# A two-chunk-first order for the attention preprocessing of a fused mixer and MLP kernel

## The chip, the cores and the metric

The kernel runs on one core of one Trainium2 chip. The metric is the device time of one execution in microseconds; several executions are timed and the median is quoted. The engines are called PE (TensorE), DVE (VectorE), ACT (ScalarE), POOL (GpSimd) and SP (SyncE, which here only issues DMAs). Each runs its own program strictly in order and waits on semaphores.

## The reference

Three stages follow each other. The first is linear attention with a complex decay per feature, the second an MLP with a hard-swish, the third a gated MLP.

```
mag   = sqrt(a_re^2 + a_im^2);  scale = min(mag, 0.999) / (mag + 1e-6)
S[t]  = a[t] * scale[t] * S[t-1] (complex) + k[t] (outer) v[t]
y[t]  = q[t] . Re(S[t])                          # 4 batches, 8 heads, 768 tokens, 48 features
h = y @ w_in;   g = h * clip(h + 3, 0, 6) / 6;   x2 = g @ w_out            # 3072 x 384 x 2048
out = ((x2 @ w1) * (x2 @ w2)) @ w3 @ w_out2                                # 384 x 1024 x 384
```

Everything is float32. The two MLPs use split products: each operand is written as a high part and a low part, and three matmuls replace one.

## The kernel before

**Tiling.** The 3072 tokens are cut into 24 chunks of 128 tokens, three to a unit, so there are 8 units of 384 tokens (`NU = 8`, `CPU = 3`). A batch is two units; the last of its six chunks carries no state on. The first MLP walks a unit in 16 *slots*, one per tile of 128 hidden features (`FT1 = 16`). Slot n has the matmuls of `gemm1` for hidden tile n (L796, into `hb`) and those of `gemm2` for tile n-2 (L816, into `acc`). Between them a tile goes through four engine steps: ACT adds 3 and clips below (`t_sb`, "relu", L1046), DVE forms the hard-swish (`g_sb`, L1237), ACT copies its high part (`gH`, `high_g`, L1036), POOL subtracts to get the low part (`gL`, L1328). `g_sb` and `t_sb` are single buffers, so the relu of a slot waits for the hard-swish of the slot before and the hard-swish for the low part of the slot before. Units run from -2 to 7; units -2 and -1 have no MLP and only prepare.

**What runs beside it.** While unit u is in the MLP, the attention of unit u+1 is done chunk by chunk and the decays of unit u+2 are computed. Three tables say in which slot what stands.

- `steps(u, sl)` gives the preprocessing steps `t = 0..15` of a unit p ("the chain") that ACT and DVE do in a slot; for u of 1 and more, step t of p = u+2 stands in slot t. The chain works in place on `AR`, `AI` and three work tiles `W1`, `W2`, `W3` (all 128 x 1152). It takes logarithm, magnitude, arctangent and running sums of the decays, then multiplies q and k by the exponentials of the sums ("products", L1170 and L1183, into `QKs`) and by cosine and sine ("rotation", L1198 into `QKc`, L1202 into `QKs`).
- `chunk(u, sl, stage)` gives the attention. In units of 1 and more, TK (transposes of k, L832) stands in slots 1, 5, 9, S (scores, L846) in 2, 6, 10, and YU (the output y and the state product, L865 to L878) in 4, 8, 12. After TK, ACT and DVE copy k out (L1059 to L1061, L1249 to L1251). After S, DVE masks the scores (L1260). After YU, ACT takes y's high part (L1067), DVE its low part (L1266) and adds to the state `Z` (L1218, L1221), decaying it for the next chunk (L1228).
- `W3_COPY`, `SPLIT_H` and `SPLIT_L` place the copies of the product w3 times w_out2 and the splitting of the first MLP's weights in the early units.

**SP's queue.** All transfers but five are issued by SP, in program order. `load_a` (L640) fetches `AR` and `AI` for the next p. `load_q` and `load_k` (L651, L656) fetch q and k for all three chunks of p. `scatter_pair` (L338 to L342; "sorting") moves the rotated rows of the first two chunks from `QKc` and `QKs` into head order in `F`, five DMAs for each source; `scatter_last` (L670) does it for the third chunk, once the first chunk's YU has freed the buffer. `store_x` (L707 to L712) sends y as the MLP's input `xHL`, in six DMAs, after DVE's low part of y. For p = 0 ACT issues the second five DMAs of `scatter_pair`.

Within a slot, the order on an engine matters below. ACT: relu, (in slot 1 the two copies L409 of the previous unit's result), the chain's step, `high_g`, the copies after TK, y's high part. DVE: hard-swish, the chain's step, the copies after TK, masks, y's low part and the state. SP: `scatter_last`, `load_v`, `store_x`, `load_q`, `load_k`, then what the chain's step asks for (`load_a` at t = 12, `scatter_pair` at 14 and 15).

At the end of unit 7 the second MLP's weights are split, each in one piece: ACT's copies in slots 4, 6, 8 (L1081), DVE's subtractions in 5, 7, 9 (L1279). After the last unit comes the second MLP (L937, L959), which the change does not touch.

## Time and profile before

| | us |
|---|---|
| median of the timed runs (3) | 1017.98 |
| lowest and highest of them | 1017.22 and 1024.38 |
| the profiled execution's own time | 1022.37 |
| its span, first to last instruction | 1020.6 |
| PE busy in the span | 910.4 |
| DVE, ACT, POOL busy | 470.5, 430.5, 256.6 |

The span is what the profile shows; 1.8 us lie around it. Units 0 to 7 of the first MLP run from about 101 us to 707 us. PE's busy time is nearly the span, so what counts are the places where it idles and the stretches in which its clock is low. A slot can be followed by ACT's relu (L1046): one stands in each slot, 128 in all.

### The profile page before, as it was taken

What the parts mean: (1) busy time and instruction counts of PE and PEld (TensorE: products, weight loads), DVE (VectorE), ACT (ScalarE), POOL (GpSimd) and SP (SyncE); (2) the same over time, 40 slices, a digit from 0 to 9 for tenths busy, and PEclk for the clock granted to TensorE, in tenths of its full rate; (3) what the DMA queues carried; (4) which work ended last, traced back from release to release, by engine and by line L of the source; (5) the groups of instructions that cost most, each with busy time, mean ns of one, the idle gap of its engine ahead of it and who ended that gap; (6) DMA issues with size and microseconds to landing.
All of it is one profiled execution on the core that took longest, in us unless ns stands there. A gap on an engine that the chain in (4) does not pass through costs nothing.

```text
span 1020.6 us, 14665 instructions
## 1 busy us (share of the span) xinstructions
PE 910.4 (89%) x5721; PEld 834.9 (82%) x5721; DVE 470.5 (46%) x610; ACT 430.5 (42%) x650; POOL 256.6 (25%) x200
## 2 busy tenths in 40 slices
PE   6944469889989989989989989989999999999996
PEld 3534468879889889889889889989888888888886
DVE  6445549849658648648748733233212121212110
ACT  4543535555655655555555532353212122212121
POOL 1011336222222222222222222343222222222221
PEclk9977769989989999999999999999999999999999
DMA  9584132353343343343344141510101010101000
GB/s 347 201 230 128 46 63 78 85 119 88 108 87 95 100 91 98 93 90 99 107 89 110 48 84 50 188 68 11 44 1 62 1 62 1 62 1 62 1 32 33
DMA packets 73688, 85.85 MB, mean 84 GB/s; under 512 B 6928, under 2 KB 59792, under 8 KB 73616
## 3 DMA queue, kind: packets, MB, share of 16 engines
q1 hardware_dynamic: 73216, 84.07, 29.7%
q10 hardware_dynamic: 400, 0.80, 0.5%
q8 instruction: 48, 0.79, 0.3%
q14 instruction: 24, 0.20, 0.1%
HBM read 45.22 MB, written 11.01 MB: 55 GB/s over the span
## 4 chain that ended last, share of the span: by engine, by line
issue 39%; PE 38%; POOL 14%; DVE 3%; ACT 2%; DMA 2%; SPq 1%; ACTq 0%; POOLq 0%; DVEq 0%
POOL gL L1328 13%; PE hb L937 10%; PE acc L959 7%; PE bQ L937 5%; PE bR L937 5%; PE bP L959 2%; PE hb L796 2%; PE acc L816 2%; PE acc L890 2%; DMA F<-QKs 1%; PE hb L890 1%; DVE QKc L1198 1%; DMA wo_sb<-in_moe_w_out_dram 1%; PE bQ L846 0%; PE bR L846 0%
## 5 line engine op out<-in xcount | busy, mean ns | idle before, releaser
L1328 POOL TENSOR_TENSOR gL<-g_sb,gH 128x384 fp32r<-128x384 f32 x128 | 157.1, 1227 | 428.2 <-ACT gH L1036 425.9
L796 PE MATMUL hb<-xHL,winH 128*128 128x384 f32 x768 | 168.6, 356 | 10.7 <-DMA xHL<-yHL 9.1
L816 PE MATMUL acc<-gH,woutH 128*128 128x384 f32 x384 | 134.0, 349 | 32.5 <-POOL gL L1328 23.6
L1237 DVE SCALAR_TENSOR_TENSOR g_sb<-t_sb,hb 128x384 f32<-128x384 f32 x128 | 70.4, 550 | 189.6 <-ACT t_sb L1046 105.8
L796 PEld LDWEIGHTS hb<-xHL,winH 128*128 128x128 f32 x768 | 140.2, 199 | 13.3 <-DMA xHL<-yHL 9.5
L1046 ACT ACTIVATE t_sb<-hb,cst 128x384 f32<-128x384 f32 x128 | 74.4, 581 | 154.1 <-PE hb L796 153.4
L816 PE MATMUL acc<-gH,woutL 128*128 128x384 f32 x384 | 133.3, 347 | 0.0
L816 PE MATMUL acc<-gL,woutH 128*128 128x384 f32 x384 | 132.8, 346 | 0.0
L1341 POOL TENSOR_TENSOR pL<-p_sb,pH 128x512 fp32r<-128x512 f32 x48 | 67.0, 1396 | 231.9 <-ACT pH L1098 231.9
L816 PEld LDWEIGHTS acc<-gH,woutH 128*128 128x128 f32 x384 | 75.0, 195 | 37.6 <-issue 29.3
L1036 ACT CAST gH<-g_sb 128x384 fp32r<-128x384 f32 x128 | 65.3, 510 | 79.4 <-DVE g_sb L1237 79.2
L796 PE MATMUL hb<-xHL,winL 128*128 128x384 f32 x384 | 88.9, 339 | 0.0
L816 PEld LDWEIGHTS acc<-gH,woutL 128*128 128x128 f32 x384 | 75.4, 196 | 0.0
L816 PEld LDWEIGHTS acc<-gL,woutH 128*128 128x128 f32 x384 | 75.2, 196 | 0.0
L1090 ACT COPY a_sb<-hb 128x512 f32<-128x512 f32 x48 | 28.1, 586 | 102.7 <-PE hb L937 102.7
L796 PEld LDWEIGHTS hb<-xHL,winL 128*128 128x128 f32 x384 | 70.4, 192 | 0.0
L1296 DVE TENSOR_TENSOR p_sb<-a_sb,bQ 128x512 f32<-128x512 f32 x24 | 16.5, 688 | 110.2 <-PE bQ L937 94.4
L1098 ACT CAST pH<-p_sb 128x512 fp32r<-128x512 f32 x48 | 29.8, 621 | 85.5 <-DVE p_sb L1296 85.5
L1296 DVE TENSOR_TENSOR p_sb<-a_sb,bR 128x512 f32<-128x512 f32 x24 | 16.5, 686 | 104.7 <-PE bR L937 99.7
L846 PE MATMUL bQ<-F 128*128 128x128 f32 x192 | 32.5, 323 | 28.2 <-DMA F<-QKs 26.8
L846 PEld LDWEIGHTS bQ<-F 128*128 128x128 f32 x192 | 29.3, 228 | 31.9 <-DMA F<-QKs 29.7
L959 PE MATMUL acc<-woH,pL 128*128 128x384 f32 x144 | 48.7, 338 | 0.0
(148 smaller groups left out, 1715.9 us busy)
## 6 DMA issues: line engine op xcount, KB each, us to landing
QKs<-in_qk_x_dram SPq DMA_DIRECT2D x16, 576.0 KB, 4.2
xHL<-yHL SPq DMA_DIRECT2D x48, 144.0 KB, 2.7
F<-QKc SPq DMA_DIRECT2D x16, 292.5 KB, 4.7
AR<-in_a_re_x_dram SPq DMA_DIRECT2D x8, 576.0 KB, 3.9
AI<-in_a_im_x_dram SPq DMA_DIRECT2D x8, 576.0 KB, 4.8
v_sb<-in_v_dram SPq DMA_DIRECT2D x24, 192.0 KB, 2.5
x_dram<-x_sb SPq DMA_DIRECT2D x24, 192.0 KB, 4.1
out_dram<-o_sb SPq DMA_DIRECT2D x6, 768.0 KB, 4.3
```

The lines of the kernel that those rows point to most:

```text
L796: mm = pe.matmul(o, w[:, kk * DF1 + ft * P:kk * DF1 + (ft + 1) * P], xv(u)[:, 2 * kk + part, :], start=(i == 0), stop=(i == 8))
L816: mm = pe.matmul(acc[m][:, 0:UNIT], w[:, ft * DM + m * P:ft * DM + (m + 1) * P], gg[:, (n % 3) * UNIT:(n % 3 + 1) * UNIT], start=(ft == 0 ...
L846: mm = pe.matmul(bk[:, hh * P:(hh + 1) * P], qk(f_of(g))[:, b, P:2 * P], qk(f_of(g))[:, b, 0:P], start=True, stop=True)
L890: mm = pe.matmul(w3_banks[i % nb][:, 0:DM], w3t_sb[:, j * DF2 + i * P:j * DF2 + (i + 1) * P], wo2_sb[:, j * DM:(j + 1) * DM], start=(j == ...
L937: mm = pe.matmul(bk[n % 2][:, :], w[:, kk * DF2 + ft * P:kk * DF2 + (ft + 1) * P], x[:, o:o + UNIT2], start=(i == 0), stop=(i == 8))
L959: mm = pe.matmul(acc2[tb][:, 0:DM], pp[:, o:o + P], w[:, ft * DM:(ft + 1) * DM], start=(ft == 0 and i == 0), stop=(ft == FT2 - 1 and i == 2))
L1036: act.copy(gH[:, (n % 3) * UNIT:(n % 3 + 1) * UNIT], g_sb[:, :]).then_inc(s["hswish_high"], 1)
L1046: act.activation(t_sb[:, :], hb[n % 2][:, 0:UNIT], ACT.Relu, bias=THREE_C).then_inc(s["relu_done"], 1)
L1237: dve.scalar_tensor_tensor(out=g_sb[:, :], in0=t_sb[:, :], scalar=6.0, in1=hb[n % 2][:, 0:UNIT], op0=ALU.min, op1=ALU.mult).then_inc(s["hs ...
L1296: dve.tensor_tensor(p_sb[:, (n % 2) * UNIT2:(n % 2 + 1) * UNIT2], a_sb[:, (n % 2) * UNIT2:(n % 2 + 1) * UNIT2], bb[n % 2][:, :], ALU.mult) ...
L1328: pool.tensor_tensor(gL[:, (n % 3) * UNIT:(n % 3 + 1) * UNIT], g_sb[:, :], gH[:, (n % 3) * UNIT:(n % 3 + 1) * UNIT].bitcast(F32), ALU.subt ...
L1341: pool.tensor_tensor(pL[:, (n % 3) * UNIT2:(n % 3 + 1) * UNIT2], p_sb[:, (n % 2) * UNIT2:(n % 2 + 1) * UNIT2], pH[:, (n % 3) * UNIT2:(n % ...
```

## The change

It rewrites the chain's last steps and moves several others.

- q and k are loaded in two pieces, chunks 0 and 1 of a unit (`load_pair`, issued at TK of the second chunk) and chunk 2 (`load_last`, at TK of the third), where it was q and then k.
- Products and rotation are done for the two first chunks (t = 10 and t = 12) and later for the third (t = 13 and t = 14). Six full-width instructions become twelve: six of two thirds, six of one third.
- DVE's sums move from t = 7 and 11 to t = 6 and 9, the arctangent's product from 8 to 7. ACT's exponentials and arctangent stand together at t = 8 (were 9 and 10), the turns at 10 (was 12), sine and cosine with their table loads at 11 (was 13).
- ACT's `high_g` stands ahead of the chain's step in a slot (and ahead of the copies L409), where it stood behind it.
- `scatter_pair` is issued at t = 12, both halves, and always by SP; `load_a` at t = 13, waiting for the last products.
- The tables of the early units move: the w3 copies earlier or later, the weight splits in another order, and the chain's steps of units 1 and 2 by one slot.
- The second MLP's weights are split in six halves, in slots 3 to 8 (ACT) and 4 to 9 (DVE), and their loads are issued two slots earlier.

```diff
-                return ([(1, 0)] if sl == 0 else []) + ([(1, sl + 1)] if sl < 9 else [])
+                return {0: [(1, 0), (1, 1)]}.get(sl, [(1, sl + 1)] if sl < 10 else [])
...
-            return [(u + 2, sl)] if u + 2 < NU else []
+            if u == 1 and sl < 2:
+                return [(3, 0), (3, 1)] if sl else []
+            return [(u + 2, sl)] if u + 2 < NU and sl < 15 else []
...
-                    sp.wait_ge(s["k_decayed"], p)
+                    sp.wait_ge(s["last_decayed"], 2 * p)
...
                     for p, t in steps(u, sl):
-                        if t == 12 and p + 1 < NU:
+                        if t == 12:
+                            scatter_pair(sp, p, 0)
+                            scatter_pair(sp, p, 1)
+                        if t == 13 and p + 1 < NU:
                             load_a(p + 1)
-                        if t == 14:
-                            scatter_pair(sp, p, 0)
-                        if t == 15 and p > 0:
-                            scatter_pair(sp, p, 1)
...
                         act.activation(t_sb[:, :], hb[n % 2][:, 0:UNIT], ACT.Relu,
                                        bias=THREE_C).then_inc(s["relu_done"], 1)
+                        high_g(n)
                         if sl == 1 and u > 0:
                             evac_x2_act(act, u - 1)
-                    if n is not None:
                         for p, t in steps(u, sl):
                             pre(p, t)
-                        high_g(n)
...
+                if t == 12:
+                    dve.wait_ge(s["pair_decayed"], 2 * (p + 1))
                     dve.wait_ge(s["cos_turns"], p + 1)
                     for i in range(2):
-                        dve.tensor_tensor(part(QKc, i), part(QKs, i), tokens(W3), ALU.mult).then_inc(s["cos_rotated"], 1)
-                if t == 15:
+                        dve.tensor_tensor(pair(part(QKc, i)), pair(part(QKs, i)), pair(tokens(W3)), ALU.mult).then_inc(s["pair_cos"], 1)
                     dve.wait_ge(s["sin_turns"], p + 1)
                     for i in range(2):
-                        dve.tensor_tensor(part(QKs, i), part(QKs, i), tokens(W2), ALU.mult).then_inc(s["sin_rotated"], 1)
+                        dve.tensor_tensor(pair(part(QKs, i)), pair(part(QKs, i)), pair(tokens(W2)), ALU.mult).then_inc(s["pair_sin"], 1)
+                if t == 13:
+                    dve.wait_ge(s["last_dma"], 16 * (p + 1))
+                    for i, grow in enumerate((AI, AR)):
+                        dve.tensor_tensor(last(part(QKs, i)), last(part(QKs, i)), last(tokens(grow)), ALU.mult).then_inc(s["last_decayed"], 1)
...
-                    if u == NU - 1 and sl in (4, 6, 8):
-                        i = sl // 2 - 2
+                    if u == NU - 1 and 3 <= sl < 9:
+                        i, part2 = divmod(sl - 3, 2)
                         act.wait_ge(s[f"mlp2_w_dma{i}"], 16)
-                        act.copy(w2parts[i][0][:, :], w2parts[i][2][:, :]).then_inc(s["mlp2_w_high"], 1)
+                        act.copy(half(w2parts[i][0], part2), half(w2parts[i][2], part2)).then_inc(s["mlp2_w_high"], 1)
```

**Place 1: SP at the end of a unit (u from 1 to 4).** The last DMAs of `store_x`, then what stands before the next unit. Before:

```order
L711 DMA xHL<-yHL 16x2x128
L712 DMA xHL<-yHL 16x2x128
L640 DMA AR<-in_a_re_x_dram 128x1152
L640 DMA AI<-in_a_im_x_dram 128x1152
L338 DMA F_68<-QKc 48x2x780
L339 DMA F_68<-QKc 48x2x780
L340 DMA F_68<-QKc 32x2x520
L341 DMA F_68<-QKc 16x2x260
L342 DMA F_68<-QKc 16x2x260
L338 DMA F_68<-QKs 48x2x780
```

And with the change:

```order
L722 DMA xHL<-yHL 16x2x128
L345 DMA F_68<-QKc 48x2x780
L346 DMA F_68<-QKc 48x2x780
L347 DMA F_68<-QKc 32x2x520
L348 DMA F_68<-QKc 16x2x260
L349 DMA F_68<-QKc 16x2x260
L345 DMA F_68<-QKs 48x2x780
L346 DMA F_68<-QKs 48x2x780
L347 DMA F_68<-QKs 32x2x520
L348 DMA F_68<-QKs 16x2x260
L349 DMA F_68<-QKs 16x2x260
L647 DMA AR<-in_a_re_x_dram 128x1152
```

The ten DMAs of `scatter_pair` have moved from behind the loads of `AR` and `AI` to ahead of them.

**Place 2: ACT in slots 8 to 10 of such a unit, chunk 1's y among them** (`W_63`, `W_64`, `W_65` are `W1`, `W2`, `W3`). Before, from slot 8's relu:

```order
L1046 ACTIVATE t_sb<-hb,cst 128x384
L1036 CAST gH<-g_sb 128x384
L1067 CAST yHL<-bP 128x4x128
L1046 ACTIVATE t_sb<-hb,cst 128x384
L1013 ACTIVATE AI<-AR 128x1152
L1014 ACTIVATE AR<-AR 128x1152
L1036 CAST gH<-g_sb 128x384
L1046 ACTIVATE t_sb<-hb,cst 128x384
L1017 ACT_TABLE_LOAD
L1017 ACTIVATE W_64<-W_64 128x1152
L1036 CAST gH<-g_sb 128x384
```

And with the change:

```order
L1052 ACTIVATE t_sb<-hb,cst 128x384
L1042 CAST gH<-g_sb 128x384
L1022 ACTIVATE AI<-AR 128x1152
L1023 ACTIVATE AR<-AR 128x1152
L1025 ACT_TABLE_LOAD
L1025 ACTIVATE W_64<-W_64 128x1152
L1072 CAST yHL<-bP 128x4x128
L1052 ACTIVATE t_sb<-hb,cst 128x384
L1042 CAST gH<-g_sb 128x384
```

The exponentials, the table load and the arctangent, spread over slots 9 and 10 before, now stand in slot 8 ahead of y's high part. (Before, `mid_decay`, L1010, stands between the first two rows.)

**Place 3: ACT around sine and cosine.** Before, in slots 12 and 13:

```order
L1036 CAST gH<-g_sb 128x384
L1067 CAST yHL<-bP 128x4x128
L1046 ACTIVATE t_sb<-hb,cst 128x384
L1023 ACTIVATE W_65<-W_63 128x1152
L1025 ACT_TABLE_LOAD
L1025 ACTIVATE W_65<-W_65,cst 128x1152
L1026 ACTIVATE W_64<-W_63 128x1152
L1027 ACT_TABLE_LOAD
L1036 CAST gH<-g_sb 128x384
```

And with the change, in slots 11 and 12:

```order
L1052 ACTIVATE t_sb<-hb,cst 128x384
L1042 CAST gH<-g_sb 128x384
L1031 ACTIVATE W_65<-W_63 128x1152
L1033 ACT_TABLE_LOAD
L1033 ACTIVATE W_65<-W_65,cst 128x1152
L1034 ACTIVATE W_64<-W_63 128x1152
L1035 ACT_TABLE_LOAD
L1052 ACTIVATE t_sb<-hb,cst 128x384
L1042 CAST gH<-g_sb 128x384
L1072 CAST yHL<-bP 128x4x128
```

The block of five has moved from behind the last y's high part (slot 12) to ahead of it, and the high part of its own slot now stands ahead of the block.

## Rows read from the trace of the kernel before

**Rows 1.** Page, parts 1 and 2: busy times, and the granted clock by slices.

```profile
PE 910.4 (89%) x5721; PEld 834.9 (82%) x5721; DVE 470.5 (46%) x610; ACT 430.5 (42%) x650; POOL 256.6 (25%) x200
...
PEclk9977769989989999999999999999999999999999
```

**Rows 2.** Waits of PE: engine line, released by, us in total, times, longest.

```profile
PE bQ L846 <- DMA F<-QKs: 26.8, 8, 9.1
PE acc L816 <- POOL gL L1328: 23.6, 10, 8.0
...
PE acc L816 <- ACT gH L1036: 6.9, 5, 2.1
```

**Rows 3.** Timeline of PE, stalls at the starts of units 4 and 5: start, us.

```profile
428.65 0.52 PE L816 MATMUL acc<-gH,woutH 128*128 128x384 f32 x1 [2.10 <-POOL gL L1328]
...
445.94 2.08 PE L846 MATMUL bQ<-F 128*128 128x128 f32 x8 [2.72 <-DMA F<-QKs]
...
503.35 0.41 PE L816 MATMUL acc<-gH,woutH 128*128 128x384 f32 x1 [2.37 <-POOL gL L1328]
```

**Rows 4.** Windows of 1 us at an earlier boundary: length, PE, PEld, DVE, ACT, POOL, PEclk, DMA.

```profile
293.00:294.00 1.00, 1.00 (x5) 1.00 (x4) 0.62 (x4) 0.98 (x1) 0.85 (x1) 0.50 1.06 128
298.00:299.00 1.00, 1.00 (x7) 1.00 (x6) 0.69 (x1) 0.00 (x0) 0.00 (x0) 0.50 0.08 16
```

**Rows 5.** Timeline of ACT, slots 13 and 14 of unit 4.

```profile
494.77 0.58 ACT L1046 ACTIVATE t_sb<-hb,cst 128x384 f32<-128x384 f32 x1 [1.11 <-PE hb L796]
495.52 1.17 ACT L1023 ACTIVATE W<-W 128x1152 f32<-128x1152 f32 x1 [0.16 <-DVE W L1188]
...
501.62 0.51 ACT L1036 CAST gH<-g_sb 128x384 fp32r<-128x384 f32 x1
```

**Rows 6.** Timeline of ACT in plain slots of unit 7: the pitch of slots.

```profile
656.78 0.58 ACT L1046 ACTIVATE t_sb<-hb,cst 128x384 f32<-128x384 f32 x1 [1.40 <-PE hb L796]
...
659.90 0.58 ACT L1046 ACTIVATE t_sb<-hb,cst 128x384 f32<-128x384 f32 x1 [0.29 <-PE hb L796]
```

**Rows 7.** Timeline of DVE in slot 8 of unit 4.

```profile
474.94 0.55 DVE L1237 SCALAR_TENSOR_TENSOR g_sb<-t_sb,hb 128x384 f32<-128x384 f32 x1
...
478.76 0.68 DVE L1266 TENSOR_TENSOR yHL<-bP,yHL 128x512 fp32r<-128x512 f32 x1
```

**Rows 8.** Groups by line, chain work of ACT and DVE: shapes, count, busy us, mean ns.

```profile
L1178 DVE TENSOR_TENSOR_SCAN W<-W,total,W 128x384 f32<-128x384 f32 x12 | 14.1, 1230 | 0.2 <-ACT W L1017 0.2
...
L1198 DVE TENSOR_TENSOR QKc<-QKs,W 128x1152 f32<-128x1152 f32 x16 | 28.3, 1807 | 6.9 <-ACT W L1025 6.9
...
L1017 ACT ACT_TABLE_LOAD x8 | 10.3, 1283 | 0.1
...
L1013 ACT ACTIVATE AI<-AR 128x1152 f32<-128x1152 f32 x8 | 9.3, 1162 | 1.0 <-DVE W L1146 1.0
```

**Rows 9.** Timeline, last y of unit 4's attention and SP's issues behind it.

```profile
495.60 0.68 DVE L1266 TENSOR_TENSOR yHL<-bP,yHL 128x512 fp32r<-128x512 f32 x1
...
500.27 0.53 SPq L640 DMA_DIRECT2D AR<-in_a_re_x_dram  x1
```

**Rows 10.** Timeline of SP, first and last of the ten DMAs of the pair.

```profile
432.54 0.60 SPq L338 DMA_DIRECT2D F<-QKc  x1
...
440.62 0.59 SPq L342 DMA_DIRECT2D F<-QKs  x1
```

**Rows 11.** DMA issues by line: KB each, us from issue to landing.

```profile
AI<-in_a_im_x_dram SPq DMA_DIRECT2D x8, 576.0 KB, 4.8
```

**Rows 12.** Timeline of PE, stalls before and in unit 0.

```profile
62.54 2.08 PE L846 MATMUL bQ<-F 128*128 128x128 f32 x8 [9.05 <-DMA F<-QKs]
...
123.02 0.66 PE L816 MATMUL acc<-gH,woutH 128*128 128x384 f32 x1 [8.03 <-POOL gL L1328]
```

**Rows 13.** Timeline of PE and group of ACT, the second MLP's weights in unit 7.

```profile
684.93 0.66 PE L816 MATMUL acc<-gH,woutH 128*128 128x384 f32 x1 [2.38 <-POOL gL L1328]
...
L1081 ACT CAST w2H<-w_raw 128x3072 fp32r<-128x3072 f32 x1 | 2.8, 2769 | 0.0
```

More of the change, by code:

```diff
@@ L259, in rows_of, with half @@
             return t[:, :].rearrange("p (c j n) -> p j c n", j=KT, n=QK)
+        def half(t, i):
+            n = N1 // 2
+            return t[:, i * n:(i + 1) * n]
         def hd(t):
@@ L753, in _ @@
                         load_x2(0)
-                    if u == NU - 2 and sl == 15:
+                    if u == NU - 2 and sl == 13:
                         for i in range(2):
@@ L1274, in _ @@
                             pre(p, t)
-                    if u == NU - 1 and sl in (5, 7, 9):
-                        i = (sl - 5) // 2
-                        hi, lo, raw = w2parts[i]
-                        dve.wait_ge(s["mlp2_w_high"], i + 1)
-                        dve.tensor_tensor(lo[:, :], raw[:, :], hi[:, :].bitcast(F32), ALU.subtract).then_inc(s["mlp2_w_low"], 1)
+                    if u == NU - 1 and 4 <= sl < 10:
+                        i, part2 = divmod(sl - 4, 2)
+                        hi, lo, raw = (half(w_, part2) for w_ in w2parts[i])
+                        dve.wait_ge(s["mlp2_w_high"], sl - 3)
+                        dve.tensor_tensor(lo, raw, hi.bitcast(F32), ALU.subtract).then_inc(s["mlp2_w_low"], 1)
             split_x2_dve(dve, 0)
```

117 lines of the change are left out of this document (58 added, 59 removed).

## The prediction

> **What bounds the kernel now.** I read the page first. PE is busy for 910.4 of 1020.6 us and its granted clock is full from the middle on; in the first 23 of 40 slices it dips again and again, and DVE (470.5) and ACT (430.5) are far from full over the span [rows 1]. So PE bounds, and what can be won are its idle 110 us and what the low clock adds to them. PE's waits name the causes: 26.8 us for the sorted rows of F, 23.6 for POOL's low part, 6.9 for ACT's high part [rows 2]. The timeline of PE places them. From unit 1 on they come once a unit: about 2.1 for the low part, then 2.7 for F [rows 3]; just behind such stalls the granted clock is 0.50, the 1.2 GHz level, while PE is busy the whole of each window, at one boundary from 293 to 299 [rows 4]. A unit takes 503.35 - 428.65 = 74.7 us [rows 3].
>
> The first of the two comes from ACT: in slot 13 it does its relu and then the chain's five instructions from 495.52 on, 6.1 us, before the high part at 501.62 [rows 5]. A plain slot is 659.90 - 656.78 = 3.12 us [rows 6], and a tile has two slots from hidden to its second matmul. The second comes from DVE's rotation in slots 14 and 15 and the ten DMAs behind it. Together with the clock I put a boundary's loss at 5.5 + 3.3 = 8.8 us: six windows at half clock are 3 us of lost work.
>
> **The change, part by part.** The cycle of a unit closes through one event, DVE's low part of the last y. I call its end T: 495.60 + 0.68 = 496.28 in unit 4 [rows 9]. Before, the first scores of a unit start at 445.94, T comes 50.3 later, and from T to the next first scores it is 74.7 - 50.3 = 24.4 us [rows 3, 9].
>
> *From T to the scores.* Six DMAs of `store_x` take SP from T to 500.27, 4.0 us [rows 9]. Then, with the change, come the ten DMAs of the pair, 440.62 + 0.59 - 432.54 = 8.7 us [rows 10], and only behind them AR and AI, 0.5 for the first and 4.8 from AI's issue to landing [rows 11]: T + 18.0. ACT waits for this in slot 0 of the next unit (the squares, t = 0) and holds back all behind it: two squares 2.1, the relu of slot 1 0.5, DVE's hard-swish 0.5, the high part 0.5, the copies of the old unit's result 0.9. That is T + 22.5. PE's second matmuls of the new unit need those copies, 1.6, so the scores start at T + 24.1, against T + 24.4. The wait for F itself is gone (its rows land at about T + 17.5), but a wait for AR and AI takes its place. That part gives nothing.
>
> On what the ten DMAs cost SP, the 8.7 us are this trace's. The Trainium skill, DMA: Bandwidth & Descriptors, section "Issuing engines are not separate DMA queues", says that issuing from several engines only saves the sequencer's time to initiate, "which is usually small relative to the DMA itself". Here it is not small: 8.7 us of issue against about 5 to landing. By the page AR and AI would be little behind T + 9, the squares would wait for nothing, and about 8 us a unit would come off; I go by the row.
>
> *From the scores to T.* Three things come later. (1) Sine and cosine with their two table loads now stand in slot 11, behind that slot's high part but ahead of slot 12's relu. From their start: 6.1 [rows 5], relu 0.5, hard-swish 0.55 [rows 7], the pair's rotation, 4 instructions at two thirds of 1.81 [rows 8] = 4.8, y's low part 0.7: T is 12.6 later. With slot 11's high part on its own time (slot 13's relu at 494.77 [rows 5], less two slots of 3.1 and 5.1, plus 1.6: 488.1) T would be 500.7: 4.5 later than 496.28. (2) But it won't be on time. DVE's running sums, 3 x 1.23 [rows 8] and 1.3 for centring, move ahead of slot 6's masks, and make slot 8's hard-swish about 1.8 late. In slot 8 ACT now does two exponentials (2.1), a table load (1.28) and the arctangent (1.2), 4.6 us [rows 8], ahead of y's high part, while DVE stands at y's low part. That starts 0.55 + 0.5 + 4.6 + 0.6 = 6.2 behind the hard-swish, at 474.94 + 1.8 + 6.2 = 483.0; it was at 478.76 [rows 7], so 4.2 late. (3) From there DVE has no gap: 1.8 for y and the state, 0.55, the other sums 4.1, 0.55, the pair's products and the rounding 5.0, masks 1.4, 0.55, and ACT's high part 0.5: 497.4 in place of 488.1. T is then 497.4 + 12.6 = 510.0, 13.7 late. I take 11.5 a unit, since each link was taken at its full length, with 4.2 (nothing late but (1)) and 14 as ends. In the slots from 9 to 16 PE stalls in pieces: for the masks (2 us), for slot 12's hard-swish (3 to 4), for slot 13's behind the rotation (2), for the input `xHL` (1 to 2); in odd units slot 9's transposes wait for the state (up to 4).
>
> So the high part's own move wins the 2.1 us that it is meant to, and the chain behind it costs more. Four units (1 to 4) have both ends of this: 4 x 11.5 = +46. Unit 5 has no load of AR and AI behind it; T is 12 late, but the scores start when F has landed and PE has got there, T + 17.5 rather than T + 24.4: +5 (ends -3 and +8).
>
> *The early part.* The rotated pair of p = 0 is done some 5.5 us earlier, because the arctangent no longer stands behind a w3 copy. SP alone issues its ten DMAs, 4.4 us more than two queues side by side, and AR and AI for p = 1 come behind them, so the first scores' 9.05 us wait [rows 12] shrinks but masks wait for the chain: unit 0 begins 0 to 5.5 us earlier, I take 3. In unit 0 the stall of 8.03 us for the high part [rows 12] falls to about 5 (the chain still sits before the next relu), and the rotation is a slot earlier; I take 9.5 by slot 5, less 2.5 at the start of unit 1, where AR and AI are late again. Together -10, ends -20 and 0.
>
> *Unit 7.* The copies of 2.77 us become halves of 1.4, which fit in a slot of 3.12 beside 1.1 of relu and high part [rows 6, 13]. Slots 3 to 15 last 44.1 us where 12 x 3.12 = 37.4 are due; the 2.38 us stall is one of three [rows 13]. I take -5.5, ends -6.7 and 0.
>
> Splitting six instructions in twelve costs nothing to speak of: one third by itself is 0.55 as the hard-swish of the same width [rows 7], three of them 1.65 against 1.81 [rows 8].
>
> *Sum.* 46 + 5 - 10 - 5.5 = +35.5 on the profiled execution's 1022.4 us (span 1020.6 and 1.8 around it) is 1057.9. The median of the runs is 4.4 lower, so 1053.5; I say 1053.
>
> **The rivals.**
>
> *DVE keeps up.* If ACT's block in slot 8 falls in time that DVE has to spare (it is busy for under half of the span [rows 1], and some gap stands in each slot before), only (1) is left: 4 x 4.2 = 17, unit 5 about -3, and -15.5 for the early part and unit 7: -1.5, that is 1016. What decides is whether y's low part in slot 8 starts within 1 us of where it did. Against it: DVE's gaps in the middle of a unit before are about 9 of 44 us, and ACT's block alone takes half of them.
>
> *It does what it looks meant to.* AR and AI arrive in time, F's rows too, and the high part never waits. That would be if SP gets to the pair's DMAs early, ahead of `store_x`'s wait; for it speaks that F's wait is the largest row [rows 2] and that the rotation is two slots earlier. Against it: in SP's order the pair stands behind the last `store_x`, so an earlier rotation alone brings nothing. Price: 5 boundaries x 8.8 = -44, the early part -18, unit 7 -5.5: 950; with half of the boundaries' gain and the early part as forecast 980. It decides if T comes no later than before and AR and AI land within 10 us of it.
>
> *Worse.* The same mechanism with the low clock on top: PE stalls of 2 to 4 us follow each other from slot 9 to slot 2 of the next unit, and half clock over 10 us more in each of four units is 5 us each, with the early part at its bad end: 1053 + 20 + 10 = 1083. It decides if the clock stays at 0.5 in most of these slots.
>
> **How the numbers follow.** Forecast (1030 to 1075) 0.52, DVE keeps up (1003 to 1024) 0.18, as meant (945 to 1000) 0.22, worse 0.08. A measurement of this kernel tells about 1% from no change, 10 us. As meant is all faster; of the second case 0.04 is faster, 0.11 within 1%, 0.03 slower; the forecast and the worse case are slower. That gives faster 0.26, same 0.11, slower 0.63. The range leaves out the worse case and a little over half of the third case: 985 to 1077; the forecast's own range is 1030 to 1075.
>
> **What would show it.** In the new trace: AR's issue about 12.7 us behind the last y's low part, and in ACT's timeline the squares ending its longest idle time, on the load; PE waiting for `acc`'s copies or `Kc` at the start of units 2 to 5, no longer for F; y's high part in slot 8 starting right behind the arctangent, and DVE idle there for 5 us; units of about 86 us between first scores, against 74.7; unit 7 with no stall over 1 us. Wrong would be units under 74 us, squares that wait for nothing, or DVE idle in slots 9 to 11.

## The result and the profile after

| | before | changed | ratio (95% interval) |
|---|---|---|---|
| median of 4 runs each, us | 1017.6 | 1091.55 | 1.071 (1.066 to 1.076) |
| span of the profiled execution, us | 1020.6 | 1090.0 | |

The changed kernel is 7% slower, 74 us. The forecast had the sign and about half of the size (+35.5), and the measured time lies outside its range.

The page of the changed kernel, parts 1 and 2, the same rows as [rows 1]:

```profile
PE 925.9 (85%) x5721; PEld 846.0 (78%) x5721; DVE 483.6 (44%) x661; ACT 431.2 (40%) x653; POOL 254.3 (23%) x200
...
PEclk9966889869979988898987999999999999999999
```

PE has the same 5721 matmuls as before, so its 15.5 us more are the lower clock: there are more slices below 9 than in [rows 1], and they reach further, to slice 22 where it was 12. The other 54 us are idle time of PE. Its waits (engine line, released by, us in total, times, longest), against [rows 2]:

```profile
PE acc L826 <- ACT x_sb L416: 44.5, 5, 11.8
PE bQ L856 <- ACT Kc L1066: 22.8, 3, 12.9
PE hb L806 <- DVE g_sb L1249: 22.6, 10, 5.6
...
PE bQ L856 <- DMA F<-QKs: 6.3, 2, 5.5
...
PE acc L826 <- POOL gL L1340: 1.0, 1, 1.0
```

Both large rows of before are gone, F's from 26.8 to 6.3 and the low part's from 23.6 to 1.0. Larger ones stand in their place: five times PE waits for ACT to empty `acc`. The waits of all engines say what ACT and DVE are waiting for:

```profile
ACT gH L1042 <- DVE g_sb L1249: 205.4, 128, 6.7
DVE g_sb L1249 <- ACT t_sb L1052: 203.7, 51, 15.2
...
ACT W L995 <- DMA AI<-in_a_im_x_dram: 67.9, 8, 12.0
DVE yHL L1278 <- ACT yHL L1072: 47.4, 16, 5.7
```

The first row turned out to be the one that I had not thought of. Before, the first two read:

```profile
DVE g_sb L1237 <- ACT t_sb L1046: 105.8, 49, 8.6
...
ACT gH L1036 <- DVE g_sb L1237: 79.2, 82, 4.1
```

ACT now waits for DVE in every one of the 128 slots, where it did in 82. DVE waits for ACT about as often as before, 51 times, but for twice as long.

**A ruler for all runs.** ACT does one relu in each of the 128 slots. In its timeline the starts of the relus of slots 3 and 15 cut a unit in two: inside (slots 3 to 15) and boundary (slot 15 to slot 3 of the next unit, which holds the first scores; T lies ahead of slot 15's relu, by 8 to 9 us in the kernel before and by 3.4 to 4.0 in the changed one). For unit 3 of the changed kernel:

```profile
419.22 0.58 ACT L1052 ACTIVATE t_sb<-hb,cst 128x384 f32<-128x384 f32 x1 [1.87 <-PE hb L806]
...
480.77 0.58 ACT L1052 ACTIVATE t_sb<-hb,cst 128x384 f32<-128x384 f32 x1
...
508.56 0.58 ACT L1052 ACTIVATE t_sb<-hb,cst 128x384 f32<-128x384 f32 x1 [1.32 <-PE hb L806]
```

That is 61.6 inside and 27.8 at the boundary. Read so from the profile of each kernel (u0 is unit 0; "inside" and "boundary" are means over units 1 to 4; all in us):

| kernel | u0 slot 3 at | u0 inside | u0 to u1 | inside | boundary | u5 to u6 | u7 inside |
|---|---|---|---|---|---|---|---|
| before | 124.7 | 73.7 | 27.3 | 53.8 | 21.1 | 20.9 | 44.1 |
| changed | 128.0 | 82.6 | 28.9 | 60.9 | 29.0 | 16.6 | 37.5 |
| e1_a_ahead | 128.8 | 82.6 | 28.8 | 60.9 | 23.0 | 16.8 | 37.4 |
| e2_y_ahead | 129.0 | 85.0 | 31.0 | 59.8 | 25.8 | 15.6 | 37.4 |
| e5_both | 128.6 | 85.9 | 25.0 | 60.1 | 19.9 | 14.9 | 37.5 |
| e6_old_split | 124.1 | 84.5 | 28.4 | 61.0 | 28.9 | 16.8 | 37.5 |
| e8_early | 127.1 | 80.4 | 27.7 | 61.0 | 28.8 | 16.7 | 37.4 |
| e7_late_high | 127.6 | 77.0 | 29.0 | 57.0 | 28.8 | 16.8 | 37.4 |
| e12_ahead_late_high | 127.6 | 79.0 | 29.5 | 57.1 | 22.5 | 16.8 | 37.4 |
| e10_three | 128.5 | 84.0 | 25.6 | 60.2 | 19.3 | 15.6 | 37.5 |
| e14_spread | 127.0 | 77.1 | 29.1 | 55.1 | 18.8 | 20.5 | 37.4 |
| e15_spread_all | 127.0 | 70.0 | 27.6 | 55.1 | 18.8 | 18.9 | 37.5 |
| e16_spread_all_split | 123.7 | 69.6 | 26.7 | 55.1 | 18.7 | 20.3 | 37.5 |
| e3_before_high_first | 126.8 | 77.0 | 28.6 | 57.4 | 20.2 | 21.3 | 45.7 |
| e18_high_13 | 126.7 | 73.6 | 27.1 | 54.3 | 20.1 | 20.7 | 45.6 |
| e4_before_u7 | 126.7 | 73.3 | 27.2 | 53.8 | 20.3 | 21.1 | 37.4 |

A unit is 15.0 us longer: 7.1 inside, 7.9 at the boundary. Cut at T instead, it is 11.9 up to T and 3.2 behind it. Unit 0 and what is ahead of it lose 13.8 (3.3 + 8.9 + 1.6), unit 5 with its boundary 2.6, and the last unit wins 6.6. The pieces were taken apart one by one. The ruler has an error of its own: e4_before_u7 is the kernel before in all that runs ahead of unit 6's end, and yet its unit 0 is 2.0 us later and its boundary 0.8 shorter.

### The profile page after: what moved, and what is told of

Same layout as the page of the kernel before. It is cut to its first block, busy times and chain, and to the rows that moved or that the text cites. A ratio compares the mean times of both kernels' runs of the same rounds, so it can differ in the third digit from the quotient of the medians.

```text
span 1090.0 us, 14722 instructions
## 1 busy us (share of the span) xinstructions
PE 925.9 (85%) x5721; PEld 846.0 (78%) x5721; DVE 483.6 (44%) x661; ACT 431.2 (40%) x653; POOL 254.3 (23%) x200
## 3 DMA queue, kind: packets, MB, share of 16 engines
q1 hardware_dynamic: 64400, 84.87, 28.4%
## 4 chain that ended last, share of the span: by engine, by line
PE 48%; DVE 16%; issue 13%; SPq 8%; ACT 7%; DMA 6%; POOL 2%; DVEq 0%; ACTq 0%; POOLq 0%
PE hb L947 9%; PE acc L969 7%; PE acc L826 7%; PE hb L806 7%; DMA AI<-in_a_im_x_dram 5%; PE bR L947 4%; PE bQ L947 4%; PE bP L969 2%; SPq L347 2%; DVE g_sb L1249 2%; PE acc L900 2%; POOL gL L1340 2%; DVE W L1143 1%; DVE W L1126 1%; PE bQ L856 1%
## 5 line engine op out<-in xcount | busy, mean ns | idle before, releaser
L1340 POOL TENSOR_TENSOR gL<-g_sb,gH 128x384 fp32r<-128x384 f32 x128 | 152.9, 1194 | 497.5 <-ACT gH L1042 467.9
L806 PE MATMUL hb<-xHL,winH 128*128 128x384 f32 x768 | 173.4, 363 | 31.7 <-DVE g_sb L1249 22.6
L826 PE MATMUL acc<-gH,woutH 128*128 128x384 f32 x384 | 134.7, 351 | 45.6 <-ACT x_sb L416 44.5
L806 PEld LDWEIGHTS hb<-xHL,winH 128*128 128x128 f32 x768 | 140.7, 201 | 39.4 <-DVE g_sb L1249 26.8
L1042 ACT CAST gH<-g_sb 128x384 fp32r<-128x384 f32 x128 | 65.7, 513 | 205.4 <-DVE g_sb L1249 205.4
L806 PE MATMUL hb<-xHL,winL 128*128 128x384 f32 x384 | 91.9, 349 | 0.0
L806 PEld LDWEIGHTS hb<-xHL,winL 128*128 128x128 f32 x384 | 73.2, 200 | 0.0
```

The lines of the kernel that those rows point to most:

```text
L806: mm = pe.matmul(o, w[:, kk * DF1 + ft * P:kk * DF1 + (ft + 1) * P], xv(u)[:, 2 * kk + part, :], start=(i == 0), stop=(i == 8))
L826: mm = pe.matmul(acc[m][:, 0:UNIT], w[:, ft * DM + m * P:ft * DM + (m + 1) * P], gg[:, (n % 3) * UNIT:(n % 3 + 1) * UNIT], start=(ft == 0 ...
L1042: act.copy(gH[:, (n % 3) * UNIT:(n % 3 + 1) * UNIT], g_sb[:, :]).then_inc(s["hswish_high"], 1)
L1340: pool.tensor_tensor(gL[:, (n % 3) * UNIT:(n % 3 + 1) * UNIT], g_sb[:, :], gH[:, (n % 3) * UNIT:(n % 3 + 1) * UNIT].bitcast(F32), ALU.subt ...
```

## Experiments

Each ratio is to the kernel before in runs on the same chip. "Cost" is the difference of two such ratios, times 1020 us. The ratio of the changed kernel is known to 0.005, so each cost that starts from it can be 5 us off. The spans of the profiled executions, 1090.0 us for the changed kernel, stand beside the large ones; they give somewhat less.

### The boundary: AR and AI behind the scatter

DVE, SP, ACT and PE at the end of unit 3 of the changed kernel (SP's six sends of y and the DMAs between the first and the last of the ten are left out). The last y's low part ends at T = 476.07 + 0.68 = 476.75:

```profile
476.07 0.68 DVE L1278 TENSOR_TENSOR yHL<-bP,yHL 128x512 fp32r<-128x512 f32 x1
```

```profile
480.74 0.60 SPq L345 DMA_DIRECT2D F<-QKc  x1
...
488.20 1.11 SPq L349 DMA_DIRECT2D F<-QKs  x1
489.41 1.34 SPq L647 DMA_DIRECT2D AR<-in_a_re_x_dram  x1
490.80 0.43 SPq L647 DMA_DIRECT2D AI<-in_a_im_x_dram  x1
```

```profile
496.86 1.16 ACT L995 ACTIVATE W<-AI 128x1152 f32<-128x1152 f32 x1 [10.72 <-DMA AI<-in_a_im_x_dram]
...
500.58 0.86 ACT L416 ACTIVATE x_sb<-acc 128x384 f32<-128x384 f32 x2
```

```profile
501.70 0.66 PE L826 MATMUL acc<-gH,woutH 128*128 128x384 f32 x1 [10.53 <-ACT x_sb L416]
...
504.71 1.36 PE L856 MATMUL bQ<-F 128*128 128x128 f32 x8
```

AR is issued at T + 12.7 (12.2 to 12.7 in units 1 to 4), the squares start at T + 20.1, PE goes on at T + 25.0, the scores follow at T + 28.0. PE's stall of 10.5 us is followed by half clock, shown by a window (length, PE, PEld, DVE, ACT, POOL busy, granted clock, DMA share, GB/s):

```profile
501.00:504.00 3.00, 2.30 (x7) 2.33 (x8) 2.48 (x6) 2.00 (x8) 1.72 (x1) 0.50 0.55 197
```

The experiment e1_a_ahead issues the load first:

```diff
-                        if t == 12:
+                        if t == 13:
+                            if p + 1 < NU:
+                                load_a(p + 1)
                             scatter_pair(sp, p, 0)
                             scatter_pair(sp, p, 1)
-                        if t == 13 and p + 1 < NU:
-                            load_a(p + 1)
```

> The changed kernel with one move in SyncE's order: AR and AI of the next unit are issued ahead of the pair's ten scatter DMAs instead of behind them. In the changed kernel ACT's squares start 20.1 us after the last y's low part (T), and the first scores 25.0 us after T. Theory (the load stands behind the scatter on SyncE and decides the start of a unit): AR and AI land at about T + 10, the squares wait for nothing there, the rows of F decide instead at about T + 18.5; 5 boundaries x 6.4 = -32 us, and a few us of clock, so 1050 to 1062. Rival (the chain inside the unit is late, the boundary only shows it): the wait changes its name and the time falls by less than 10 us, 1082 to 1092. A second rival: AR and AI now delay the ten scatters and the rows of F land later, T + 22: -15 us, about 1076.

Measured: 1065.4 us, ratio 1.043 (1.041 to 1.045), a cost of 28.6 us by the ratios and 23.4 by the spans. The boundary falls by 6.0, the inside by nothing, as the theory has it. The total is 3 us short of its interval, because only the boundaries of units 1 to 4 fall (4 x 6.0 = 24) and the one behind unit 0, the theory's fifth, does not. The wait of the squares is nearly gone (13.2 us in all where it was 67.9), and PE waits for F instead (43.7 for 6.3):

```profile
477.40 1.17 ACT L995 ACTIVATE W<-AI 128x1152 f32<-128x1152 f32 x1 [1.47 <-DMA AI<-in_a_im_x_dram]
```

```profile
487.63 1.16 PE L856 MATMUL bQ<-F 128*128 128x128 f32 x8 [3.57 <-DMA F<-QKs]
```

With T at 465.88 + 0.68 = 466.56 the scores start at T + 21.1. The second rival has some truth too: the rows of F land later. Part 6 of the page (KB each, us from issue to landing), of the changed kernel and then of this one:

```profile
F<-QKc SPq DMA_DIRECT2D x16, 292.5 KB, 4.7
F<-QKs SPq DMA_DIRECT2D x16, 292.5 KB, 5.7
...
AI<-in_a_im_x_dram SPq DMA_DIRECT2D x8, 576.0 KB, 7.2
```

```profile
F<-QKc SPq DMA_DIRECT2D x16, 292.5 KB, 7.9
F<-QKs SPq DMA_DIRECT2D x16, 292.5 KB, 7.2
...
AI<-in_a_im_x_dram SPq DMA_DIRECT2D x8, 576.0 KB, 6.5
```

So the same ten DMAs, 8.6 us of issue here, decide what stands behind them. By the sentence of the Trainium skill that the forecast weighed (DMA: Bandwidth & Descriptors, "Issuing engines are not separate DMA queues": the issue is "usually small relative to the DMA itself") this order would hardly matter; the runs disagree, by 23 to 29 us.

### Inside and around T: blocks ahead of y

ACT in slot 8 of unit 4 of the changed kernel, then DVE, which needs y's high part:

```profile
534.89 1.16 ACT L1022 ACTIVATE AI<-AR 128x1152 f32<-128x1152 f32 x1
...
537.13 1.28 ACT L1025 ACT_TABLE_LOAD   x1
538.42 1.17 ACT L1025 ACTIVATE W<-W 128x1152 f32<-128x1152 f32 x1
539.50 0.57 ACT L1072 CAST yHL<-bP 128x512 fp32r<-128x512 f32 x1
```

```profile
540.09 0.69 DVE L1278 TENSOR_TENSOR yHL<-bP,yHL 128x512 fp32r<-128x512 f32 x1 [5.66 <-ACT yHL L1072]
```

This is the 4.6 us block of the forecast, and DVE idle for 5.7 beside it. The experiment e2_y_ahead turns the order within those slots:

```diff
 # ACT
-                            pre(p, t)
+                            if t != 8:
+                                pre(p, t)
...
                         act.copy(yv(0), ...).then_inc(s["y_high"], 1)
+                    for p, t in steps(u, sl):
+                        if n is not None and t == 8:
+                            pre(p, t)
 # DVE: the same for t = 10 and 12, behind y's low part and the state
```

> The changed kernel with the order within slots changed: ACT's two exponentials, table load and arctangent (4.6 us) go behind y's high part in their slot, and DVE's rounding and rotation (t = 10 and 12) go behind the masks and y's low part of theirs. Theory (these blocks stand ahead of work that PE waits for, and make T late): T comes 3 to 6 us earlier in each of units 1 to 4 and the time is 1068 to 1080. Rival (the chain itself is the long line and T is set by sine, cosine and the rotation whatever stands beside them): the masks and y are earlier, the rotation later, T as before: 1086 to 1097. Worse (the arctangent is later by a slot's wait, and DVE's sums behind it too): 1100 to 1110.

Measured: 1075.5 us, ratio 1.053 (1.050 to 1.055), a cost of 18.8 us by the ratios and 14.3 by the spans. It is as the theory said: T comes 4.0 to 4.8 us earlier behind slot 3's relu, since the rotation no longer stands ahead of the last y, and the ruler shows as much, 3.2 at the boundary and 1.1 inside. Unit 0 with its start and boundary is 5.5 longer in turn. In slot 8 little is won. DVE's idle 5.7 us ahead of y in slot 8 became 1.1, but it stood 3.3 us for the next slot's relu, which was now behind the block:

```profile
529.41 0.69 DVE L1283 TENSOR_TENSOR yHL<-bP,yHL 128x512 fp32r<-128x512 f32 x1 [1.07 <-ACT yHL L1073]
...
534.48 0.56 DVE L1253 SCALAR_TENSOR_TENSOR g_sb<-t_sb,hb 128x384 f32<-128x384 f32 x1 [3.32 <-ACT t_sb L1052]
```

A block of 4.6 us on an in-order engine in a slot of 3 to 6 us has to stand ahead of something.

> Both moves together: AR and AI ahead of the pair's scatter, and the chain's blocks behind y's parts in their slots. If the two costs add (the boundary behind T, and T itself): 1091.5 - 35 - 17 = about 1040, from 1028 to 1050. If both take from the same slack: no more than the better one of the two alone, 1055 or above.

Measured: 1049.35 us, ratio 1.0275 (1.026 to 1.029): 44 us less than the changed kernel, against 28.6 + 18.8 = 47, or 41.4 against 23.4 + 14.3 = 37.7 by the spans. Within the noise they add.

### The high part's own move

Here the forecast claimed a gain of 2.1 us a unit. The edit alone, in the kernel before:

```diff
                        act.activation(t_sb[:, :], ...).then_inc(s["relu_done"], 1)
+                        high_g(n)
                         ...
                             pre(p, t)
-                        high_g(n)
```

> The kernel before with one line moved: ACT's high part stands ahead of the chain's step in its slot, as in the changed kernel. Theory (PE's stall of about 2.1 us a unit behind slot 13's five chain instructions goes, and the same block then stands ahead of nothing that PE needs so soon): 5 units x 2 = -10 us against the kernel before, from -4 to -16, so a ratio of 0.984 to 0.996. Rival (the chain's step is late by the wait for the relu's hard-swish, and everything behind it with it: rotation, scatter, F): 0 to +10 us, ratio 1.000 to 1.010.

Measured: 1043.3 us, ratio 1.022 (1.019 to 1.025): 23 us slower. And the reverse, in the changed kernel:

> The changed kernel with the high part back behind the chain's step in its slot. Theory (the move by itself is good in either kernel: without it POOL's low part and PE wait for the blocks of 4.6 and 6.1 us): 4 to 16 us slower than the changed kernel, 1095 to 1108. Rival (the move holds the chain back, and that is part of what made the changed kernel slow): 5 to 15 us faster, 1076 to 1087.

Measured: 1066.0 us, ratio 1.045 (1.041 to 1.049): 26 us faster than the changed kernel. Both expectations called this the rival, and both sizes are beyond what it was given. The stall that the move was meant to remove does go: in the kernel before with this edit alone, PE's wait for the low part falls from 23.6 to 6.2 us. But its waits for the hard-swish and for the copies of the old unit's result rise, from 1.6 to 20.2 and from nothing to 13.1. The inside falls from 60.9 to 57.0, and rises from 53.8 to 57.4 in the kernel before. The timelines show how. First ACT before, slots 12 and 13 of unit 3:

```profile
414.21 0.58 ACT L1046 ACTIVATE t_sb<-hb,cst 128x384 f32<-128x384 f32 x1 [1.40 <-PE hb L796]
...
417.46 0.51 ACT L1036 CAST gH<-g_sb 128x384 fp32r<-128x384 f32 x1 [0.55 <-DVE g_sb L1237]
...
420.35 0.58 ACT L1046 ACTIVATE t_sb<-hb,cst 128x384 f32<-128x384 f32 x1 [1.89 <-PE hb L796]
420.83 1.16 ACT L1023 ACTIVATE W<-W 128x1152 f32<-128x1152 f32 x1
```

Then the same with the high part first:

```profile
427.01 0.58 ACT L1046 ACTIVATE t_sb<-hb,cst 128x384 f32<-128x384 f32 x1 [1.21 <-PE hb L796]
430.46 0.51 ACT L1036 CAST gH<-g_sb 128x384 fp32r<-128x384 f32 x1 [2.87 <-DVE g_sb L1237]
...
433.15 0.59 ACT L1046 ACTIVATE t_sb<-hb,cst 128x384 f32<-128x384 f32 x1 [0.64 <-PE hb L796]
435.79 0.51 ACT L1036 CAST gH<-g_sb 128x384 fp32r<-128x384 f32 x1 [2.05 <-DVE g_sb L1237]
436.21 1.16 ACT L1023 ACTIVATE W<-W 128x1152 f32<-128x1152 f32 x1
```

and DVE there:

```profile
429.89 0.54 DVE L1237 SCALAR_TENSOR_TENSOR g_sb<-t_sb,hb 128x384 f32<-128x384 f32 x1
432.08 0.76 DVE L1186 TENSOR_SCALAR W<-W 128x1152 f32<-128x1152 f32 x1 [1.65 <-ACT W L1020]
```

The high part needs the hard-swish, which DVE does only behind its own long chain work. With the high part in front, ACT stands idle for it (2.9 and 2.1 us in these two slots), and only then starts the chain's step, for which DVE in turn waits. Before, ACT did that step while DVE was busy. Sine and cosine start 3.1 us behind their slot's relu (436.21 - 433.15) instead of 0.5. Of the waits, ACT's for the hard-swish is 79.2 us before, 204.4 with this one edit, 205.4 in the changed kernel, and 112.0 in it with the edit undone.

Is it slot 13 with the long block, where I expected the gain, or the other slots? The edit for slot 13 alone; e19_high_rest has the opposite condition:

```diff
                        act.activation(t_sb[:, :], ...).then_inc(s["relu_done"], 1)
+                        if u > 0 and sl == 13:
+                            high_g(n)
                         ...
                             pre(p, t)
-                        high_g(n)
+                        if not (u > 0 and sl == 13):
+                            high_g(n)
```

> The kernel before with the high part ahead of the chain's step in slot 13 of units 1 to 7 only, where sine, cosine and two table loads (6.1 us) stand. Theory (the gain of the move is there, its cost in the other slots, where ACT now stands for the hard-swish before it starts the chain's step and DVE then waits for ACT): PE's stall of 2.1 us in slot 14 goes, the rotation comes 1.5 to 2 later; -8 to +2 us, ratio 0.992 to 1.002. Rival (the cost is made in slot 13 as well, through the later rotation and rows of F): +5 to +12 us, 1.005 to 1.012.

> The kernel before with the high part ahead of the chain's step in all slots but slot 13 of units 1 to 7. Theory as above: the whole cost of the move, +20 to +30 us, ratio 1.020 to 1.030. Rival: half of it, +8 to +16, 1.008 to 1.016.

Measured: slot 13 alone 1024.4 us, ratio 1.003 (1.001 to 1.005); the rest alone 1038.1, ratio 1.018 (1.015 to 1.021). Both lie just between what the two theories gave. Four fifths of the cost (18 of 22 us) are made in the other slots, but slot 13 has no gain either: PE's wait for the low part falls from 23.6 to 16.3 us, but that for ACT's high part rises from 6.9 to 10.5.

### The last unit

> The kernel before with the last unit's part of the change alone: the second MLP's weights are split in halves over six slots, and loaded two slots earlier. In the changed kernel slots 3 to 15 of unit 7 took 37.5 us in place of 44.1. Theory (this part is independent of the rest): -6.6 us, from -5 to -8, ratio 0.992 to 0.995. Rival (it only came through because all else was late by then and the loads had longer to land): 0 to -2 us, ratio 0.998 to 1.000.

The edit is the change's own last unit, put in the kernel before:

```diff
-                    if u == NU - 1 and sl in (4, 6, 8):
+                    if u == NU - 1 and 3 <= sl < 9:
+                        i, part2 = divmod(sl - 3, 2)
...
-                    if u == NU - 2 and sl == 15:
+                    if u == NU - 2 and sl == 13:
```

Measured: 1013.5 us, ratio 0.992 (0.989 to 0.995): -8 us. Unit 7's inside is 37.4 where it was 44.1 (12 plain slots are 37.4), so 6.7 of it are seen there. A weight has two copies of 1.5 us now where it had one of 2.77 [rows 13], the first of them:

```profile
669.38 1.48 ACT L1085 CAST w2H<-w_raw 128x1536 fp32r<-128x1536 f32 x1
```

> The kernel before with both parts: high part ahead of the chain's step, and the last unit's halves. If each does by itself what is expected and they add: -10 - 6.6 = -16.6 us, ratio 0.984 (0.978 to 0.990). If the high part's move gives nothing: -6.6, ratio 0.9935.

Measured: 1035.1 us, ratio 1.015 (1.012 to 1.018). Neither of the two expected values, since both took the high part for a gain; the measured parts add: +22 - 8 = +14, and it is +16.

### The early part

The edits, in the changed kernel, of e6_old_split and of e8_early:

```diff
-        ORDER_W = (0, 1, 4, 2, 5, 3, 6, 7)
-        SPLIT_W = {(-2, 15): (0,), (-1, 3): (1,), ...
+        ORDER_W = (0, 4, 1, 5, 2, 6, 3, 7)
+        SPLIT_H = {(-1, 0): (0,), (-1, 8): (4,), ...
+        SPLIT_L = {(-1, 1): (0,), (-1, 8): (4,), ...
```

```diff
-                        15: [(2, 12), (2, 13), (2, 14)]}.get(sl, [(2, sl - 3)])
+                        3: [(2, 0), (2, 1)], 15: [(2, 13), (2, 14)]}.get(sl, [(2, sl - 2)])
```

> The changed kernel with the old kernel's order and slots of splitting the first MLP's weights. Theory (in the early part DVE instructions with two SBUF inputs stand while GpSimd subtracts, 3.4 to 3.8 us each, and the new slots put these on the chain and the rotation): 8 to 20 us less, 1071 to 1083, all of it before unit 1's fourth slot. Rival (the early part is late because AR and AI land late there too, and the splits only fill gaps): within 4 us, 1087 to 1095. It would be slower, 1095 to 1105, if the new order of the weights is what lets unit 0 begin as early as it does.

Measured: 1088.15 us, ratio 1.065 (1.063 to 1.067), 6 us less by the ratios, whose intervals overlap, and 2.7 by the spans, so a small gain at most: the time is the rival's. Unit 0's slot 3 is 3.9 us earlier, but its inside 1.9 longer. The mechanism of the theory exists and is shown below, but it is a small part of the 24 us by which the early part was missed.

> The changed kernel with that last edit alone: in unit 0 the chain of unit 2's tokens one slot earlier. Same theory: 4 to 9 us less than the changed kernel, 1082 to 1087. Rival: within 3 us, 1088 to 1094.

Measured: 1087.0 us, ratio 1.064 (1.061 to 1.068): 7 us less by the ratios, 4.5 by the medians, but the intervals overlap. The ruler agrees in the place (u0 inside 80.4 for 82.6, the next boundary 27.7 for 28.9).

### Adding up, and what was left

These combine the edits above: load, blocks and high part (e10_three), load and high part, and all three with that of e8_early.

> The changed kernel with three moves together: AR and AI ahead of the pair's scatter, the chain's blocks behind y's parts in their slots, and the high part back behind the chain's step. Alone they gave -28, -19 and -25 us against the kernel before of their own job, the first two together -44. Theory (three costs that add): +73 - 28 - 19 - 25 = about 0 against the kernel before, 1012 to 1028. Rival (with the high part back, the chain is no longer late, so the second move has nothing left to win, or they share it): 1030 to 1045.

> The changed kernel with two moves: AR and AI ahead of the pair's scatter, and the high part back behind the chain's step. If they add: +73 - 28 - 25 = +20 against the kernel before, about 1039. If T now comes so early that the rows of F or the load decide all the same: +30 to +40, about 1053.

> The three moves and, in unit 0, the chain of unit 2's tokens one slot earlier (t = slot - 2 as before, in place of slot - 3, so that slot 15 has two steps and not three). Theory (in the changed kernel slots 11 to 15 of unit 0 take 28.7 us where they took 16.3, since the whole tail of that chain meets there): 4 to 9 us less than with the three moves alone. Rival (these blocks cost the same wherever they stand): within 3 us of it.

Measured: all three 1047.6 us, ratio 1.026 (1.023 to 1.029), the rival and 3 us above its interval; load and high part alone 1040.7, ratio 1.019 (1.016 to 1.022), within 2 us of what adding gives; with unit 0's chain a slot earlier 1044.3, ratio 1.023 (1.019 to 1.026), inconclusive against 1047.6. So once the high part is back, putting the blocks behind y costs 7 us instead of winning 14 to 19. In units 1 to 4 it is even: the inside is 60.2 with it and 57.1 without, the boundary 19.3 and 22.5. The ruler finds 2 us of the loss in unit 0 and 2 in unit 5, whose boundary wins back only 1.2; the spans of the two profiled executions differ by 4.4. What stayed were 3.3 us inside, 1.4 at the boundary, and unit 0. For that, the chain's steps were put back in their old slots, with the loads by chunks, products and rotation in two parts and sorting by SyncE left as changed (on top of the high part's return):

```diff
-            return [(u + 2, sl)] if u + 2 < NU and sl < 15 else []
+            ts = {8: (), 9: (8,), 10: (), 11: (9,), 12: (10,), 13: (11, 13), 14: (12,), 15: (14,)}.get(sl, (sl,))
+            return [(u + 2, t) for t in ts] if u + 2 < NU else []
```

The last chunk's products (t = 13) fall in slot 13, where in the kernel before DVE is idle for 6.8 us during sine and cosine, and SP's load of AR and AI then comes ahead of the scatter by itself. For the second of the three, unit 0 got the same (the third adds e6_old_split's tables):

```diff
-                        15: [(2, 12), (2, 13), (2, 14)]}.get(sl, [(2, sl - 3)])
+                        3: [(2, 0), (2, 1)], 10: [], 11: [(2, 8)], 12: [], 13: [(2, 9)], 14: [(2, 10)],
+                        15: [(2, 11), (2, 13), (2, 12), (2, 14)]}.get(sl, [(2, sl - 2)])
```

> The changed kernel with the high part back behind the chain's step, and from unit 1 on the chain spread over the slots as in the kernel before: the arctangent's step in slot 9, the sums in 11, sine and cosine in 13 together with the last chunk's products, the pair's rotation in 14, the last's in 15. SyncE then issues AR and AI in slot 13, ahead of the pair's DMAs. Theory (what is left of the loss is where the chain's blocks stand, slots 3 to 15 at 57.6 against 54.4 and the boundary at 20.8 to 23.8 against 21): units 1 to 4 take 54.4 within and 19 to 21 at the boundary, 18 to 26 us less than the two-move version of 1041, so 1014 to 1022, a ratio of 0.995 to 1.003. Rival (the sorting by SyncE alone and the loads by chunks cost by themselves): 1027 or above.

> The same, with the chain of unit 2's tokens in unit 0 spread as before too. Theory (the early part is late by the same blocks: slots 3 to 15 of unit 0 took 73.7 us before, 82.6 with the change, 77.0 with only the high part back): 3 to 7 us less than with units 1 to 4 alone spread, about 1012. Rival: within 2 us of it.

> The same again, with the old slots for splitting the first MLP's weights as well. Theory (as in the run of the splits alone): 1 to 4 us less, about 1009, and with the last unit's halves in it below the kernel before by 1%. Rival: no difference that can be told.

| kernel | us | ratio (95%) |
|---|---|---|
| e14_spread | 1018.7 | 0.998 (0.997 to 1.000) |
| e15_spread_all | 1009.65 | 0.9885 (0.985 to 0.992) |
| e16_spread_all_split | 1006.35 | 0.985 (0.982 to 0.988) |

The first and the third are within what the theory gave, the second won 9 us where 3 to 7 were given. The places of the blocks in the slots are the rest of the loss, from unit 1 on (1.0188 - 0.9981, 21 us) and in unit 0 (10 us). Which block's place counts for how much was not tried. The last version beats both kernels: 1.5% below the one before, 8% below the changed one, though its gain over e15_spread_all is within the intervals. By the ruler it is 15.7 us ahead of the kernel before at unit 7's slot 15: 6.7 of it are the last unit's halves, 5.7 unit 0 with its start and boundary, and 4 the boundaries of units 1 to 4 less a longer inside. So it keeps a part of the change that is good. The boundary is 18.7 against 21.1 (20.3 in e4_before_u7), where only two thirds of the rotation stand ahead of the scatter; that this is the reason was not tried by itself.

## Why the forecast was right in sign and wrong in size

- **Scores to T.** Taken as 11.5 us later, with 4.2 and 14 as ends. From slot 3's relu to T it is 11.9 longer in each of units 1 to 4 (57.6, 57.0, 57.6, 57.0 for 45.6, 45.1, 45.7, 45.1). The 4.6 us block, DVE idle beside it and the sine block are all there as worked out, but that the size came out is in part luck: 3.9 of the 11.9 belong to the high part's move, which the forecast had as a gain (with it undone, T comes 53.7, 53.0, 53.7 and 52.9 behind slot 3). What it did price comes to 8 us, not 11.5.
- **First step that failed, "That part gives nothing"** (T to the scores). The mechanism was right: a wait for AR and AI takes the place of that for F, and AR is issued at T + 12.7, as forecast to the tenth. Too small was what follows: the squares start at T + 20.1, not at T + 18.0. AI is issued 1.4 us behind AR where 0.5 was taken, and the squares start 6.1 us behind that issue where 4.8 was taken from [rows 11]; the load now runs behind ten DMAs of F. The scores start at T + 28.0, not T + 24.1; 2.1 of it is this, 1.4 that PE needs 3.0 us from its restart to the scores, at half clock, and not 1.6. From T to the next slot 3 it is 3.1, 3.2, 1.6 and 4.8 us longer in units 1 to 4. That makes the units 15.0 longer each, and 4 x 3.5 = 14 us of the miss.
- **Second step that failed, the early part: -10 forecast, +13.8 measured.** That is 24 us of the miss. The forecast had unit 0 begin 3 us earlier, win 9.5 more by slot 5, and lose 2.5 at the start of unit 1; what lies between it put at nothing. By the starts of the relus, unit 0 begins 2.9 us later and is 1.0 earlier in slot 5. From there to unit 1's first slot it loses 5.9, and 9.0 in the first three slots of unit 1. (Of these, what happens up to slot 5 is near the ruler's error of 2 us; the rest is clear of it.) The first scores' wait did shrink (from 9.05 to 5.5 us) and so did the stall of 8.03 us (to 5.6, now for the hard-swish; forecast 5). But in slot 3 of unit 0 PE stands longest, 12.9 us, for copies that ACT does behind the squares, and these for AI behind the ten DMAs:

```profile
142.78 2.05 PE L856 MATMUL bQ<-F 128*128 128x128 f32 x8 [12.86 <-ACT Kc L1066]
```

The order of the loads is not enough to get this back: with AR and AI ahead, PE stands 13.5 us there for F, and unit 0's inside stays 82.6. What the experiments do take off it: 5.6 is again the high part's move (82.6 to 77.0 when undone), and another 7 is where the chain's steps stand (77.1 to 70.0). The lateness that I worked out for units 1 to 4 was not applied to unit 0, which has the same blocks and three steps in its slot 15.
- **Third step that failed, beneath both: "the high part's own move wins the 2.1 us that it is meant to".** It costs 3.6 to 3.9 us a unit inside, 23 to 26 us in all, in either kernel. I had looked only at slot 13, where a long block stands in the way of a part that is ready, and not at the other slots, where the part isn't ready and blocks the chain. [rows 5] shows the sine block starting 0.16 us behind DVE's step for it: there ACT had no time to spare ahead of the block.
- **Unit 5** +2.6, forecast +5: 6.9 longer inside, 4.3 shorter at the boundary, where no load stands. **Unit 7** -6.6, forecast -5.5, and -8 alone.
- **The rivals.** "DVE keeps up" asked for y's low part in slot 8 within 1 us; DVE stood for it for 5.7. "As meant" asked for AR and AI within 10 us of T; it was 20 for the second of them. "Worse" lies nearest in time (1083), but it asked for a clock of 0.5 in most of slots 9 to 2 of the next unit. The windows of unit 3's slots 9 to 15 and of the boundary behind them show 0.84 and 0.80 (the granted clock is the third number from the right):

```profile
450.60:480.80 30.20, 26.95 (x186) 26.35 (x187) 21.83 (x35) 14.40 (x24) 6.00 (x6) 0.84 0.17 45
480.80:508.60 27.80, 17.27 (x96) 16.94 (x96) 8.32 (x15) 10.94 (x19) 6.14 (x5) 0.80 0.54 123
```

Over units 1 to 4 such windows show 0.84 to 0.94 and 0.76 to 0.80. Over the span the clock fell from 0.946 to 0.920, and it rises again when an order is undone (0.937 with the load ahead): a part of the excess, not its origin.
- **Misread rows.** The forecast has the clock dip "in the first 23 of 40 slices"; [rows 1] has the last dip in slice 12. It calls the stall of 8.03 us one for the high part; [rows 12] names POOL's low part. And from 294 to 296 PE was not busy all the time (0.74 and 0.01 us of the two windows, which [rows 4] leaves out). The sum uses none of the three.

Against the sum of +35.5: 14 + 24 - 3.5 (units 5 and 7) = 34.5 more, +70; the spans differ by 69.4.

Not tried: loads of AR and AI by another engine's queue, and double buffers for `t_sb` and `g_sb`, with which ACT and DVE might wait less for each other.

## What to carry to other kernels

Before an instruction is moved ahead on an in-order engine, ask in every place it will stand whether its input is ready by then; if not, its wait becomes the wait of all behind it, and of the engine that feeds it. A critical block and a wait for an engine in the same slot belong in that order: block first, if the other engine is busy meanwhile. And DMAs that one engine issues, here 0.6 to 1.4 us each, delay what stands behind them in its program.
